# Moving ScalarE's weight rounding and VectorE's Newton step within the windows of a gated linear attention kernel with two MLP layers

## The reference

```
f = 1 / (1 + exp(-f_logit))
state = f[t] * state + outer(k[t], v[t]);   y[t] = q[t] @ state
h = x @ w_in;   g = h if h >= 1, 0 if h <= -1, else (h + 1)**2 / 4;   x1 = g @ w_out
h = x1 @ w_in2; g = (a0 + a1 h + a2 h^2 + a3 h^3) / (1 + |b0||h| + |b1|h^2 + 1e-6);   out = g @ w_out2
```

## Time and profile before

| what | value |
|---|---|
| median of three runs | 908.0 us |
| profiled execution, its own time | 907.93 us |
| its span | 906.1 us |
| PE busy | 885.0 us (98%) |
| DVE busy | 663.2 us (73%) |
| ACT busy | 631.6 us (70%) |
| POOL busy | 272.3 us (30%) |
| granted TensorE clock | 1.0 of full |

### The profile page before, as it was taken

How to read it: one execution, slowest core, us unless ns; L and a number is a source line. 1 busy time by engine, 2 the same in 40 slices (tenths; PEclk the granted TensorE clock), 3 DMA queues, 4 the chain that set the end, 5 groups by cost and what they waited for, 6 DMA issues and landing times.

```text
span 906.1 us, 13158 instructions
## 1 busy us (share of the span) xinstructions
PE 885.0 (98%) x4786; PEld 731.4 (81%) x4786; DVE 663.2 (73%) x816; ACT 631.6 (70%) x822; POOL 272.3 (30%) x200
## 2 busy tenths in 40 slices
PE   4899999999999999999999999999999999999997
PEld 3788888888888888888888887888888888888886
DVE  8877756655565655554344799999889889899885
ACT  6767565556555555554577788888787887888873
POOL 3466300010000000010055476644254244353331
PEclk9999999999999999999999999999999999999999
DMA  8652121112112311200233111001001001000001
GB/s 214 196 165 73 36 86 46 36 35 88 37 36 66 91 36 35 88 10 1 88 103 124 53 52 36 1 35 35 2 33 35 23 12 35 35 0 0 35 0 39
DMA packets 26743, 48.70 MB, mean 54 GB/s; under 512 B 4544, under 2 KB 7616, under 8 KB 26688
## 3 DMA queue, kind: packets, MB, share of 16 engines
q1 hardware_dynamic: 26688, 47.99, 17.5%
HBM read 36.18 MB, written 9.44 MB: 50 GB/s over the span
## 4 chain that ended last, share of the span: by engine, by line
PE 82%; DVE 9%; ACT 4%; issue 4%; POOL 1%; POOLq 0%; DMA 0%; DVEq 0%; SPq 0%; ACTq 0%
PE acc L1236 19%; PE acc L1187 18%; PE h_pair L1170 17%; PE at_pair L1209 10%; PE h_pair L1209 10%; PE at_pair L1110 2%; DVE growth L871 2%; PE at_pair L1129 2%; PE at_pair L1124 2%; DVE g L942 1%; ACT t L661 1%; ACT t L664 1%; DVE x_lo L935 1%; DVE t L986 1%; PE at_bank L1094 1%
## 5 line engine op out<-in xcount | busy, mean ns | idle before, releaser
L559 POOL TENSOR_TENSOR g_lo<-g,g_hi 128x1024 fp32r<-128x1024 f32 x46 | 111.0, 2413 | 212.6 <-DVE t L986 212.6
L942 DVE SCALAR_TENSOR_TENSOR g<-h_pair,t 128x512 f32<-128x512 f32 x96 | 66.3, 691 | 146.6 <-ACT t L664 146.5
L661 ACT ACTIVATE t<-h_pair,half 128x512 f32<-128x512 f32 x96 | 66.0, 687 | 98.7 <-PE h_pair L1170 97.5
L522 POOL TENSOR_TENSOR k_s<-k_in,growth 128x512 f32<-128x512 f32 x22 | 28.8, 1310 | 290.3 <-DVE growth L871 270.6
L1170 PE MATMUL h_pair<-x_hi,w_hi 128*128 128x512 f32 x288 | 113.0, 392 | 1.6 <-DVE x_lo L935 0.9
L1236 PE MATMUL acc<-g_hi,w_hi 128*128 128x512 f32 x288 | 112.2, 389 | 0.3 <-POOL g_lo L559 0.3
L1170 PE MATMUL h_pair<-x_hi,w_lo 128*128 128x512 f32 x288 | 112.2, 389 | 0.0
L1170 PE MATMUL h_pair<-x_lo,w_hi 128*128 128x512 f32 x288 | 112.1, 389 | 0.0
L1236 PE MATMUL acc<-g_hi,w_lo 128*128 128x512 f32 x288 | 112.0, 389 | 0.0
L1236 PE MATMUL acc<-g_lo,w_hi 128*128 128x512 f32 x288 | 112.0, 389 | 0.0
L1187 PE MATMUL acc<-g_hi,w_hi 128*128 128x512 f32 x264 | 107.5, 407 | 0.0
(11 more groups left out here) (171 smaller groups left out, 2047.2 us busy)
## 6 DMA issues: line engine op xcount, KB each, us to landing
w_raw<-w SPq DMA_DIRECT2D x32, 384.0 KB, 3.6
f_in<-fC SPq DMA_DIRECT2D x48, 96.0 KB, 2.9
k_in<-kC SPq DMA_DIRECT2D x48, 96.0 KB, 2.4
q_in<-qC SPq DMA_DIRECT2D x48, 96.0 KB, 2.2
mlp_out<-o_sb SPq DMA_DIRECT2D x18, 256.0 KB, 3.2
x_raw<-mlp_out SPq DMA_DIRECT2D x6, 768.0 KB, 4.4
outT<-o_sb SPq DMA_DIRECT2D x18, 256.0 KB, 2.0
v_in<-vC SPq DMA_DIRECT2D x22, 192.0 KB, 2.6
```

The lines of the kernel that those rows point to most:

```text
L522: nc.gpsimd.tensor_tensor(k_scaled(i)[:, :], k_in[u][:, :], growth[u][:, :], ALU.mult).then_inc(k_ready, 1)
L559: nc.gpsimd.tensor_tensor(g2_lo[r][:, :, :], g2[r][:, :, :], g2_hi[r][:, :, :].bitcast(F32), ALU.subtract).then_inc(lo2_ready, 1)
L661: nc.scalar.activation(t1[n % 2][:, :], h1[n % 2], ACT.Relu, scale=0.5, bias=half[:, :]).then_inc(relu1_ready, 1)
L942: nc.vector.scalar_tensor_tensor(out=g1[n % 2][:, :], in0=h1[n % 2], scalar=1.0, in1=t1[n % 2][:, :], op0=ALU.max, op1=ALU.min).then_inc(g ...
```

## The change

On ScalarE, for steps 4 to 13, the rounding of a weight piece moves behind everything that the step has of the spline and of the recurrence: before, it stood between `spline_in` and `spline_hi` in stages 1 to 3, and behind `spline_hi` in stage 0. On VectorE, in stage 2 of every window, the two Newton instructions move from between `spline_join` and `spline_lo` to just ahead of `scale_queries`, behind `spline_lo`, `states` and, where it stands there, `rest_y`.

```diff
--- before.py
+++ after.py
@@ -813,18 +813,16 @@
                     spline_in(n)
                 if stage == 0:
                     copy_keys(i)
-                elif n <= PIECES - HEAD_PIECES:
-                    split_w1(n + HEAD_PIECES - 1)
                 if n < N1:
                     spline_hi(n)
-                if stage == 0 and n <= PIECES - HEAD_PIECES:
-                    split_w1(n + HEAD_PIECES - 1)
                 if stage == 1:
                     invert(i + 1)
                 if stage == 2:
                     round_y(i)
                 if stage == 3:
                     gate_steps(i + 2)
+                if n <= PIECES - HEAD_PIECES:
+                    split_w1(n + HEAD_PIECES - 1)
                 t = n - (N1 - TILES)
                 if t in X2_STEPS:
                     split_x2(0, X2_STEPS.index(t))
@@ -1049,8 +1047,6 @@
                 spline_join(n)
                 if stage == 0:
                     mask(i)
-                if stage == 2:
-                    newton(i + 1)
                 spline_lo(n)
                 if stage == 0:
                     scan(i + 1)
@@ -1058,6 +1054,7 @@
                     states(i)
                     if i % GROUPS == LAST:
                         rest_y(i)
+                    newton(i + 1)
                     scale_queries(i + 1)
                 if n == TILES:
                     dve.wait_ge(coef_loaded, 32)
```

## The result

The changed kernel takes 914.7 us (median of 5 runs, 913.68 to 916.2) beside 908.56 for the kernel before: a ratio of 1.0063, 95% interval 1.0045 to 1.0083, so 5.7 us slower with 4.1 to 7.5 as bounds. Its profiled execution took 913.45 us at a span of 911.7, 5.6 more than the span before.

The account below looks back on a forecast made before the run. Two near-equal loops, TensorE's and VectorE/ScalarE's, run until 112 us, then TensorE bounds. 1.25 + 1.98 + 0.73 + 0.73 - 0.75 + 0 = +3.95 on 907.93 gives 911.9 us, range 908.0 to 914.4.

Parts of the forecast that it names:

- two loops: Between 52 and 112 us: TensorE's round of four steps takes 20.57 us, the VectorE/ScalarE loop 20.40, slack 0.17 per window.
- (a): ScalarE's rounding in steps 5, 9, 13 now stands directly ahead of the next relu: 3 times 0.73, +2.2 us.
- (b): ScalarE's rounding in steps 7 and 11 now stands ahead of the next relu: 2 x 0.73, +1.5 us.
- (c): ScalarE's rounding in steps 6 and 10 delays the next relu about 0.7 us, but the join waits for VectorE anyway: 0.
- (e): VectorE's moved Newton: join to x_lo grows from 5.00 to 6.27 us, +1.27 in windows 1 and 2, 0 in 3.
- (d): VectorE's scan in steps 4, 8, 12 is less covered by GpSimd: gain 0.75 per window, -2.25 us in all.
- Window by window: Scores at 72.76 come 1.25 us late, the next 1.98 more less 0.17 slack, block 1's first matmul +3.95.
- rival 2: g_lo of steps 6, 10, 14 waits for nearly all of GpSimd's keys' product: +5.4, 913.3 us; chance 0.12.
- rival 3: VectorE's scan is not freed, piece and scan stay together, (d) = 0: +6.2, 914.1 us; chance 0.10.
- A proportional slowdown: g_lo on VectorE beside GpSimd costs 1.14 us in its new place; by the exclusive port rule 1.64.
- rival 4: Not slower: scan runs in 1.61 us away from GpSimd, 907.3 to 908.5; chance 0.25, shared with smaller losses within noise.

Follow-up runs that it names:

- one pause: Kernel before, with two more subtractions (1.4 us, result not used) on VectorE ahead of rest_y in step 7: 910.42 us, ratio 1.002.
- stage 3 back: Changed kernel with ScalarE's roundings of steps 7 and 11 back at their old place: 912.37 us, ratio 1.0046.
- run with the piece held: Changed kernel, but GpSimd holds the weight pieces of steps 6 and 10 until the scaled queries are done: 910.71 us, ratio 1.0026.
- ScalarE's half alone: Kernel before with only the weight roundings on ScalarE moved, Newton at its old place: 912.34 us, ratio 1.0043.
- two pauses: Kernel before, with four more subtractions (2.9 us, not used) on VectorE ahead of rest_y in step 7: 912.08 us, ratio 1.0041.
- VectorE's half alone: Kernel before with only Newton moved on VectorE, the roundings at their old places: 909.6 us, ratio 1.0011.
- run with the keys' product first: Changed kernel, but GpSimd multiplies the keys ahead of the weight piece in stage 1: 910.96 us, ratio 1.0026.

## Why the prediction was right, and where it was short

**The bound.** Right: two loops of nearly equal length ahead of 112 us, with 0.17 us of slack. The run with one pause shows it from the other side: what is added ahead of x_lo (1.44 us more idle time at the scores) arrives in full (1.49).

**(a), (b), the roundings of stages 1 and 3.** Priced at 0.73 each. In the changed kernel the rounding of 64.14 is followed by its relu at 64.86, and that of 77.10 by 77.82: 0.72. Putting stage 3 back took 0.72 and 0.74 off windows 2 and 3. Right.

**(c), that of stage 2.** Costs nothing at ScalarE, as said: it starts the next relu later (69.56, where it was 68.67), but that step's join, at 74.66, comes right behind x_lo. But it moves GpSimd's piece from 66.99 to 69.62, and there the step was read too narrowly: see (e).

**(d), the scan.** Forecast 0.75 saved per window, measured 3.87 - 3.08 = 0.79.

**(e), Newton.** The step that was mis-sized. Forecast 6.27 us from join to x_lo, measured 6.98. Newton's first instruction was taken at 0.72 us, from a row where it started 0.17 us ahead of GpSimd's piece; here it starts at 69.63, 0.01 behind a piece that started at 69.62, and takes 1.27. That alone is 0.59 us more from start to start. g_lo takes 1.33, 0.11 more than the 1.22 that it was read from. The second Newton and q_s were right at 1.11 and 1.10. The run with the piece held shows that GpSimd is the cause: without it Newton's first takes 0.69 at the same place. The missing 0.7 us in each of windows 1 and 2 is what separates 3.95 from the 5.4 measured. That the two starts fell 0.01 us apart was nothing that the prediction's rows could tell; what it could have done is to carry both prices, 0.72 and some 1.3.

**Window by window.** The three windows grew, by x_lo, by 1.94 (from the join of step 4), 2.68 and 0.80 us, where the prediction has 1.25, 1.98 and 0.71 (these sum to 3.94; it wrote 3.95). The weight pieces stayed ahead: TensorE waited for none of them. After 120 us nothing was lost, as said.

**The rivals.** By size the result, 5.7 more, is nearer to rival 2 (+5.4) and rival 3 (+6.2) than to the forecast. Rival 2, g_lo caught by the keys' product, was the right kind of thing at the wrong instruction. g_lo starts at 67.62, 0.51 us behind the product's start at 67.11 and not 0.1 to 0.2, so it waits only for the rest of it and ends 0.55 us behind the product. Before, that distance was also 0.55, and in ScalarE's half alone, for Newton's second (67.42 + 1.67) behind the product (66.79 + 1.74), 0.56. A proportional slowdown, for which the prediction had 1.14 us, doesn't fit: g_lo took 1.33, and the same two Newton instructions took from 0.69 up to 1.67 us here, by where they met GpSimd. The Trainium skill ("SBUF — State Buffer", "Who interferes with whom") calls the contention for the port that VectorE and GpSimd share an exclusive lock. The traces agree in kind, one of the two waiting for the other to end; the distance of 0.55 us is less than the 0.69 that the instruction takes alone, so part of it ran beside the other. Rival 3 (no gain at the scan) and rival 4 (the scan free in 1.61 us, and so not slower) fell with the scan's measured 2.96 us.

**What was not in it.** The clock. The changed kernel's idle 2.31 us ahead of the scores at 74.77 is followed by a stretch at half of full, 1.2 GHz instead of 2.4. Its windows:

```profile
76.00:78.00 2.00, 2.00 (x7) 1.55 (x6) 0.69 (x1) 1.97 (x4) 0.01 (x1) 0.50 0.39 148
...
78.00:80.00 2.00, 2.00 (x8) 1.64 (x7) 0.80 (x2) 1.69 (x4) 2.00 (x3) 0.75 0.00 0
```

In the profiled execution the next wait for x_lo hides that. In the six runs listed the mean clock is 0.994 to 0.998, and the time goes from 913.45 and 913.68 at 0.998 to 916.2 at 0.994. Where the longer runs lost their time stays open. One place is a fall behind such a wait where nothing hides it, as in the runs with two pauses and with stage 3 back. Another is the head of the program, before anything that the change touches: the profiled execution of VectorE's half alone, at a mean clock of 0.996, stood at 0.50 of full from 24 to 28 us, behind 1.56 us of idle time, and was 2.6 us late from there on. The kernel before also has such runs (0.995 to 0.998, up to 911.5 us). None of the longer runs of the changed kernel was profiled; so the clock as the source of the rest, between the 5.4 us of the trace and the medians' 6.1, is an inference.

## What to carry to other kernels

Before moving work into or out of idle time, compare the lengths of all loops that run side by side, and not the busy shares: here VectorE and ScalarE were idle for a quarter and a third of the 65 us to 112 and still had 0.17 us of slack per window of 20.57. When a producer moves, follow its consumer on the third engine, and look at what that one now runs beside. Here that took 2.4 us off the scans and put some 2.8 on other instructions, and what was missed of the latter is nearly all of the prediction's error. If a duration is read from a row, check that the neighbour which lengthens it starts on the same side of it. And when an experiment takes away an obstacle that the kernel before has too, its gain is not the share that the change brought in: ease both kernels, or subtract what was there.

## What the runs showed of the hardware

- VectorE's instructions with both inputs in SBUF were lengthened beside a GpSimd product or subtraction: one of 128x512 from 0.69 us to 0.86 up to 1.67, a scan instruction from 0.40 to 0.85. In three places, with starts at 63.69 before, 67.62 in the changed kernel and 67.42 in ScalarE's half alone, it ended 0.55 or 0.56 us behind the GpSimd instruction that it had met. Those with one input in PSUM (the join 0.69, x_lo 1.41 for two) kept their time in every trace.
- Whichever started first kept its time: Newton's first took 0.68 us from 66.82 while a piece started at 66.99, and that piece took 3.42 where the held one of 71.68 took 2.10; it took 1.27 from 69.63 beside a piece of 69.62, and that piece 3.02.
- TensorE's granted clock fell to 1.2 GHz for some 3 us behind idle times of 2.31 and 3.26 us ahead of the score matmuls of step 8, and of 1.73 ahead of those of step 12; and for some 7 us behind 1.56 us ahead of score matmuls in the head of VectorE's half alone, which came out 2.6 us late. It did not, in the executions profiled, behind 1.27, 1.81 and (the first scores with stage 3 back) 2.27 us, nor behind 2.33 us ahead of block 1 in ScalarE's half alone and 2.38 us in the run with the keys' product first. So the length of the idle time alone doesn't decide it; what does stays open. In the run with two pauses, where no later wait hid it, it cost 1.6 us.
